# Half of the first batch's decay matrices from device memory instead of TensorE

## The reference, cut to what matters

```python
for t in range(S):
    m_new = np.maximum(f_gate[:, :, t] + m, i_gate[:, :, t])
    f_stab = np.exp(f_gate[:, :, t] + m - m_new)
    i_stab = np.exp(i_gate[:, :, t] - m_new)
    m = m_new
    C = f_stab[:, :, None, None] * C + i_stab[:, :, None, None] * np.einsum('bhd,bhe->bhde', vt, kt)
    n = f_stab[:, :, None] * n + i_stab[:, :, None] * kt
    h_tilde = np.einsum('bhde,bhe->bhd', C, qt)
    nq = np.einsum('bhd,bhd->bh', n, qt)[:, :, None]
    y[:, :, t] = sigmoid(o_gate[:, :, t]) * h_tilde / np.maximum(np.abs(nq), 1.0)
```

## Time and profile before

| what | value |
|---|---|
| median of 3 runs | 456.21 us (454.49 to 457.3) |
| the profiled execution's own time | 455.49 us |
| its span, first to last instruction | 453.8 us |
| mean granted TensorE clock | 0.995 |
| busy: TensorE / its weight loads | 439.6 us (97%) / 407.6 us (90%) |
| busy: VectorE, ScalarE, POOL | 255.6 (56%), 209.1 (46%), 208.3 (46%) us |
| chain that ended last | PE 85%, DVE 5%, issue 4%, ACT 4%, DMA 1% |
| moved by DMA | 47.38 MB, mean 104 GB/s over the span |

### The profile page before, as it was taken

One profiled execution on the slowest core, in us unless ns is written; L12 is line 12 of the kernel. 1 busy time (PEld: TensorE's weight loads), 2 busy tenths in 40 slices (PEclk: granted clock), 3 DMA queues, 4 the chain that ended last, 5 costly groups with the idle time before them and its releaser, 6 DMA issues.

```text
span 453.8 us, 9518 instructions
## 1 busy us (share of the span) xinstructions
PE 439.6 (97%) x3463; PEld 407.6 (90%) x3463; DVE 255.6 (56%) x592; ACT 209.1 (46%) x517; POOL 208.3 (46%) x293
## 2 busy tenths in 40 slices
PE   8899999999999999899999999999999999999996
PEld 3588988999999989799999998899999998999996
DVE  7689865777765356776674237666665326213122
ACT  3666459666554247654552137655652213211120
POOL 7535421789886333888861204798883000000000
PEclk9899999999999999999999999999999999999999
DMA  7557990443344415434454013534310010000101
GB/s 211 195 168 217 348 263 27 119 129 111 103 131 146 127 43 166 143 92 131 124 154 143 1 44 102 150 120 142 126 61 1 1 43 2 0 1 0 46 1 43
DMA packets 36616, 47.38 MB, mean 104 GB/s; under 512 B 3356, under 2 KB 29082, under 8 KB 36570
## 3 DMA queue, kind: packets, MB, share of 16 engines
q1 hardware_dynamic: 35674, 45.76, 33.4%
q10 hardware_dynamic: 896, 1.02, 0.6%
HBM read 42.73 MB, written 4.03 MB: 103 GB/s over the span
## 4 chain that ended last, share of the span: by engine, by line
PE 85%; DVE 5%; issue 4%; ACT 4%; DMA 1%; DVEq 0%; POOL 0%; POOLq 0%; ACTq 0%
PE pC L1165 32%; PE pA L1236 7%; PE pA L1237 7%; PE pA L1238 7%; PE pS L1077 6%; PE pA L1165 5%; PE pY L1134 4%; PE pA L1240 3%; PE pA L1241 3%; PE pC L1015 2%; PE pY L1113 2%; PE pN L1089 2%; DVE gb L856 1%; PE pA L1195 1%; DMA x<-o_gate_dram 1%
## 5 line engine op out<-in xcount | busy, mean ns | idle before, releaser
L988 DVE SCALAR_TENSOR_TENSOR h_lo<-pA,h_hi 128x384 fp32r<-128x384 f32 x96 | 53.5, 557 | 147.9 <-ACT h_hi L760 147.9
L760 ACT ACTIVATE h_hi<-pA 128x384 fp32r<-128x384 f32 x96 | 46.8, 488 | 138.7 <-PE pA L1241 138.6
L1165 PE MATMUL pC<-wc_hi,h_hi 128*128 128x320 f32 x288 | 94.1, 327 | 1.1 <-DVE wc_lo L846 1.0
L1165 PE MATMUL pC<-wc_lo,h_hi 128*128 128x320 f32 x288 | 88.7, 308 | 0.0
L1165 PE MATMUL pC<-wc_hi,h_lo 128*128 128x320 f32 x288 | 88.4, 307 | 0.0
L494 POOL TENSOR_TENSOR gb<-gb,pb 128x384 f32<-128x384 f32 (+1 forms) x54 | 49.1, 909 | 63.9 <-ACT pb L628 63.4
L1236 PE MATMUL pA<-uT_hi,wc_hi 128*128 128x384 f32 x192 | 65.2, 340 | 0.3 <-DVE wc_lo L846 0.3
L1237 PE MATMUL pA<-uT_lo,wc_hi 128*128 128x384 f32 x192 | 64.7, 337 | 0.0
L1238 PE MATMUL pA<-uT_hi,wc_lo 128*128 128x384 f32 x192 | 64.3, 335 | 0.0
L1165 PEld LDWEIGHTS pC<-wc_hi,h_hi 128*128 128x128 f32 x288 | 54.0, 188 | 2.3 <-DVE h_lo L988 1.3
L1165 PEld LDWEIGHTS pC<-wc_lo,h_hi 128*128 128x128 f32 x288 | 54.2, 188 | 0.1
(11 more groups left out here) (135 smaller groups left out, 881.6 us busy)
## 6 DMA issues: line engine op xcount, KB each, us to landing
gb<-g_dram SPq DMA_DIRECT2D x18, 512.0 KB, 3.9
kv<-kvN_dram SPq DMA_DIRECT2D x24, 324.0 KB, 4.0
kd<-kT_dram SPq DMA_DIRECT2D x24, 180.0 KB
qz<-qT_dram SPq DMA_DIRECT2D x72, 60.0 KB
out_dram<-u SPq DMA_DIRECT2D x24, 160.0 KB, 1.9
qd<-qT_dram SPq DMA_DIRECT2D x20, 180.0 KB, 2.6
gq<-g_dram SPq DMA_DIRECT2D x45, 60.0 KB
wc_raw<-w_ch_dram SPq DMA_DIRECT2D x6, 384.0 KB, 6.1
```

Of the source, the lines that this page charges most:

```text
L760: nc.scalar.activation(h2[0][:, slot % 2], pA[slot % 2][:, 0:HALF], ACT.Relu).then_inc(h2_hi, 1)
L988: nc.vector.scalar_tensor_tensor(h2[1][:, slot % 2], pA[slot % 2][:, 0:HALF], 0.0, h2[0][:, slot % 2].bitcast(F32), ALU.max, ALU.subtract) ...
L1165: ins = mm(dst, a[p], b[q], start=first and n == 0, stop=last and n == 2)
```

## The change

In the first batch, the decays of chunks 3, 4 and 5 (`FIRST_LOADED` = 3) come the way that the later batches' do. `spread_decays` is left out for steps 9 to 17; the query decays are still spread by TensorE. SyncE stores G right behind the scores load of chunk 2, waits until both stores are complete, and loads the decays of chunks 3, 4 and 5, each as soon as the values product of the chunk that used the buffer is through. Loads around them change places: the rest of chunk 2 comes behind the stores, and the scores loads of chunks 3 and 4 come a place earlier relative to the rest of the chunk before. POOL masks each loaded chunk behind the scaling of the queries of the chunk before. ScalarE's `first_exps` waits for the mask and works in place in SBUF. A semaphore of its own, `first_masked`, counts these masks, and `decay_loads` counts the loads of the first batch too.

```diff
+FIRST_LOADED = 3
...
+        first_masked = sem("first_masked")
...
         def decay_loads(ba, c):
 
-            return (ba - 1) * (NC // Q) + c // Q + 1
+
+            return ba * (NC // Q) + c // Q + 1 - FIRST_LOADED // Q
...
             for n in range(4):
                 load_weight(n)
-            load_chunk(0, 2)
-            load_weight(4)
-            load_chunk(0, 3)
-            load_weight(5)
+            load_scores(0, 2)
             sp.wait_ge(g_ready, len(SEGMENTS))
             g_rows = G_row.rearrange("p (c t) -> p c t", t=L)
             sp.dma_start(g_dram[:, 0:NH, :].rearrange("c p t -> p c t"), g_rows).then_inc(g_out, 16)
             sp.dma_start(g_dram[:, NH:NH + 1, :].rearrange("c p t -> p c t"), g_rows[0:1]).then_inc(g_pad_out, 16)
-            load_chunk(0, 4)
+            load_rest(0, 2)
+            load_weight(4)
+            sp.wait_ge(g_out, 16)
+            sp.wait_ge(g_pad_out, 16)
+            load_decays(0, 3)
+            load_scores(0, 3)
+            load_decays(0, 4)
+            load_rest(0, 3)
+            load_weight(5)
+            load_scores(0, 4)
+            load_decays(0, 5)
+            load_rest(0, 4)
             load_weight(6)
             load_chunk(0, 5)
             for n in range(7, NW):
                 load_weight(n)
-            sp.wait_ge(g_out, 16)
-            sp.wait_ge(g_pad_out, 16)
             for c in range(R):
                 load_chunk(1, c)
...
                 for g in range(NG):
                     tile = gb[:, r, GH * g:GH * g + HEADS[g], :]
+                    done = g_masked if ba > 0 else first_masked
                     nc.gpsimd.affine_select(out=tile, in_=tile, compare_op=ALU.is_ge, fill=NEG, base=0,
-                                            pattern=[[0, HEADS[g]], [1, L]], channel_multiplier=-1).then_inc(g_masked, 1)
+                                            pattern=[[0, HEADS[g]], [1, L]], channel_multiplier=-1).then_inc(done, 1)
...
                     if c < NC - 1:
                         weigh(0, c)
                     scale_q(0, c)
+                    if FIRST_LOADED <= c + 1 < NC:
+                        mask(0, c + 1)
                     if c >= 3:
                         x_low(0, c - 3)
...
                 c, g = divmod(m, NG)
                 if g == 0:
                     act.wait_ge(aT_ready, segment(c))
-                    if c >= Q:
-                        act.wait_ge(y_mm, NG * (c - Q + 1))
-                act.wait_ge(g_mm, m + 1)
+                if c < FIRST_LOADED:
+                    act.wait_ge(g_mm, m + 1)
+                else:
+                    act.wait_ge(first_masked, m - NG * FIRST_LOADED + 1)
                 for j in range(HEADS[g]):
                     head = GH * g + j
-                    last = nc.scalar.activation(gb[:, c % Q, head, :], pA[m % 2][:, j * L:(j + 1) * L], ACT.Exp,
+                    tile = gb[:, c % Q, head, :]
+                    sums = pA[m % 2][:, j * L:(j + 1) * L] if c < FIRST_LOADED else tile
+                    last = nc.scalar.activation(tile, sums, ACT.Exp,
                                                 bias=aT[:, c, bass.ds(head, 1)])
                 last.then_inc(e_exp, 1)
...
                         if k < STEPS:
-                            spread_decays(k)
+                            if k < NG * FIRST_LOADED:
+                                spread_decays(k)
                             if k == 2:
                                 keep_warm(WARM_THIRD)
```

## The result

The kernel got slower by 3.3%: 470.23 us (468.76 to 472.49, six runs) against 455.62 (454.00 to 457.30, six runs beside them), ratio 1.033 [1.030, 1.036]. The prediction was 459.2, with 456.0 to 463.0 as its range, and it was wrong.

The account below looks back on a forecast made before the run. VectorE's queue was taken to bound the first batch's attention for 17.6 us. Its delay of 2.2 us, grown by 1.3 to 3.5, less 0.1 from TensorE, gave 455.5 + 3.4 = 458.9, with half the distance to the median 459.2; range 456.0 to 463.0.

Parts of the forecast that it names:

- The sum that gave 459.2: Whole kernel: profiled 455.5 us plus 3.4 of delay in the first batch's attention, plus half the distance to the median.
- TensorE falls to half clock in the stall: Rival, chance 0.20: TensorE idles 2.3 us in attention and its clock halves; 460.6 us with one dip, 462.0 with two.
- the first stall's 2.2: VectorE at the first weight split, started at 34.22 us before, waits 2.2 us for ScalarE, done at 36.45.
- TensorE's queue was full up to the stall: Argument against the half-clock rival: ahead of the earlier dip, before 12.93 us, TensorE had only small products.
- First decay load: Chunk 3's decays on SyncE's queue: issued at 26.7 us, landed at 32.0, first mask part ready at 32.5.
- Its use at 33 us leaves about 1 us: Chunk 3's moved scores load (keys and queries) goes out 0.5 us later than 26.7, with about 1 us to spare.
- the forecast's 4.4: Landing time in us taken for values issued right behind a decay load, in place of 3.3 without one.
- ScalarE's queue and VectorE's first stall: Three steps' exponentials stand ahead of the first weight split: ScalarE needs 3.94 us, done at 36.45; VectorE stalls 2.2.
- Chunks 4 and 5: Later loads in attention: second split ready at 42.4 us, covered by 0.1; third at 49.9, delay growing to 3.5.
- the forecast's second stall: VectorE at the third weight split waits about 1.4 us for ScalarE; the delay grows by 1.3.
- What goes: Nine steps' spreading products leave TensorE, 2.7 us of work; worth 0.3 at most, since only step 6's is on the chain.
- the forecast's 3.4: Delay in us at 51.57, the first dense product: 3.5 from VectorE's stalls less 0.1 given back by TensorE.

Follow-up runs that it names:

- before_with_stall: The kernel before with one added wait: step 9's scores wait for weight 5 to land, no added transfer; 475.99, 465.30, 474.64 and 466.79 us against 455.27.
- gap_filled: The kernel after with 12 fillers (TensorE products of constants that nobody reads) ahead of step 9's scores; 469.51 us against 455.27, 1.031.
- scores_first: The kernel after with SyncE issuing chunk 3's keys and queries ahead of that chunk's decays; 470.91 us, 1.035.
- splits_and_scores_early: scores_first with ScalarE's halves of the early weight splits three steps sooner, ahead of the exponentials that wait for POOL; 468.73 us against 454.67, 1.029.
- all_filled: The kernel after with 55 fillers (products nobody reads), ahead of steps 9 and 17 and behind the scores of steps 10 to 16; 462.95 us, 1.018.
- spread_kept: The kernel after with the spreading products of steps 9 to 17 put back on TensorE, their sums unused; 473.12 us, 1.040.
- loads_only: The kernel before with SyncE's new order and three decay loads that nobody reads; 470.44, 464.76, 472.29 and 458.89 us against 454.46.
- filled_lean: The kernel after with 29 fillers (products nobody reads), fewer than all_filled; 470.40, 458.48, 462.52 and 461.45 us, without the slowest 1.014.
- spread_left_out: The kernel before without the spreading products of steps 9 to 17, nothing in their place; ten runs, 452.88 to 467.52 us against 454.46, the seven lower 1.001.
- stall_filled: before_with_stall with 18 fillers (products nobody reads) on TensorE ahead of the added wait; 457.17 us against 454.67, 1.005.
- splits_early_filled: splits_and_scores_early with 33 fillers (products nobody reads) behind the scores of steps 9 to 17; 466.37, 459.90, 465.30 and 461.39 us, 1.018.

## Why the prediction was wrong, point by point

**The step that failed.** The sum that gave 459.2 has no term for the clock: it took the stage to run at full clock but for one chance in five. And the rival that had the clock, "TensorE falls to half clock in the stall", mis-sized its one term: "in a dip of 3.3 us it gets through 0.97 of a step where VectorE would have gone 1.65: 1.4 us each". The rival's mechanism was right, and so was its 3.4 us a step at half clock (measured 3.0 to 3.4 up to step 15). The length was not: the dip lasted 34 us, and with it the way from step 9 to the dense part took 12.6 us more (the table above). The 3.3 us were taken from the earlier trace rows, the only dip that the trace of before had, as if its length were a constant. In attention it is not: in *before_with_stall* one idle time of 3.90 us brought 41 us. With a dip up to the dense part the rival would have stood near 470 (estimate: 455.5, the first stall's 2.2, and nine steps at 3.36 instead of 2.0 us), and a range that held it at 0.20 could not have ended at 463.0.

**Its chance** was too low as well. "TensorE's queue was full up to the stall" counted against it; before the stall that *gap_filled* left, too, TensorE had been busy, and the clock fell all the same. The Trainium skill (TensorE: Matmul & The Clock Gate, "HAM oscillation — how this bites in real kernels") was the warning, and it spoke for the right case; the traces agree that idle times between bursts bring the fall. The Trainium skill (TensorE: Matmul & The Clock Gate, "Part 1: The HAM clock gate") puts the penalty of the ramp at a kernel's start under 1% of a typical span; that is no price for a fall in the middle, behind which the stage here ran up to 12.6 of 467 us longer (2.7%).

**First decay load.** Landed at 31.95 (24.95 + 7.0) against 32.0. The two errors cancel: it went out 1.75 us earlier than 26.7, as the whole start was earlier in this execution, and took 7.0 us instead of 5.3. The first mask ran at 32.10, in 0.47 us each (1.41 for three).

**"Its use at 33 us leaves about 1 us"**, of chunk 3's keys and queries, failed: they were in at 33.60, 6.11 us after the last issue, and TensorE, with its start 1.75 earlier and the early spreading products gone, wanted them at 31.08. I had given the new load's bytes to the decays alone, and not to what stands behind it: values of chunk 3 took 7.2 us instead of the forecast's 4.4, the weight 8.3 where the one of the same place took 4.2 before. (The values landed at 36.4, where 36.3 was forecast, but by two errors: issued 2.7 us sooner, 2.8 longer under way.) The burst's DMA share of 1.00 lasted until 36 us. This put TensorE's idle time at 31.1 us instead of 35.8, and on the queries instead of VectorE; *scores_first* shows that the total hardly depends on it (the +3.1 and +12.6 of the table became +1.1 and +15.0).

**ScalarE's queue and VectorE's first stall.** Right in kind and place: 36.64 against 36.45. The wait was 3.90 instead of 2.2, because VectorE came to it 1.5 us sooner (32.77 against 34.22) and the split was 0.2 later; as the rest of the start was 1.8 us sooner, the agreement of 36.64 is in part luck. *splits_and_scores_early* took this wait away, and the time hardly moved.

**Chunks 4 and 5.** The times at full clock agree to 0.2 us (*all_filled*, 42.32 and 49.94), but mostly by luck: the first split stood at 35.52 there, so that from it to the third it took 14.4 us and not 13.5, with fillers and longer landings in it, and the forecast's second stall, VectorE's for ScalarE at the third split, is in no trace at more than 0.24 us. Where the clock stood at 1.00 ahead of 47 us (*spread_kept*, *loads_only*, *filled_lean*), the second gap was TensorE's own, 2.2 to 2.3 us, at the state product that waits for POOL's weighting of chunk 4. In the kernel after there is no second gap: behind the fall TensorE was busy up to the dense part but for 0.14 us.

**What goes.** Right as far as the times can tell: 0.25 of 2.7 us in one trace (*spread_left_out*).

**Where the loss came from.** The loads make TensorE wait, at one of three places (queries of chunk 3; VectorE behind ScalarE's queue; values of chunk 3 or 4 behind POOL); an idle time of 2 to 4 us lets the clock fall; and attention then runs at half clock until the dense part. In the kernel before, such a stall is worth 2.5 us by itself, and 10 to 21 with the fall (*stall_filled*, *before_with_stall*). For the change itself the share is bounded only: of its 14.6 us at least 6.3 are the clock's, since with the fillers in it and no fall it stands at 8.3 (*all_filled*), and some 8 to 11 by the runs of *filled_lean* at 0.999 and 1.000. That any one of the gaps is enough is shown by taking others away; that the fall costs more than the stall is shown by the pair of stalls with and without fillers.

**What stays open.** The cost of this change at full clock was not measured free of fillers: *all_filled* bounds it above by 8.3 us, the runs of *filled_lean* at 0.999 and 1.000 stand at +4.0 and +7.0, and the one of *loads_only* at 1.000, which has the loads alone, at +4.4. All lie above the forecast's 3.4, with fillers or the spreading products in them, so it is neither confirmed nor excluded. Why the clock came back after 3.4 us in the first falls of *spread_kept* and *loads_only* and in other falls not for 20 to 41 us, is not explained either. No version of the change that was tried beats the kernel before.

## What to carry to other kernels

In a stage where TensorE has small products and little reserve, price a stall in two parts: its own length, and what the work up to the next dense stretch costs at half clock; the second was the larger one here (2.5 us without the fall, 10 to 21 with it). Don't take the length of one dip in the trace as that of the next. An added load is paid for by the transfers issued behind it on the same queue as much as by its own landing, so give each of them the longer landing and look up who wants it. And before removing work from TensorE where it is off the critical path, ask whether it was what kept the clock; here that is likely, not shown.

## What the runs showed of the hardware

- Half clock can outlast its cause by far. By the profile TensorE had no idle time any more (3.00 of 3 us in 63 to 66), and still the clock stayed at 0.50 until the dense products had run for 2.4 us. (The ends of matmuls are modelled, so that short gaps between them wouldn't show.) In the seven profiled executions in which gaps were left (the kernel after, *gap_filled*, *scores_first*, *spread_kept*, *before_with_stall*, *splits_and_scores_early*, *loads_only*) the last fall lasted 20 to 41 us and ended 2.4 to 5.1 us into the dense part. In *splits_early_filled*, with fillers in every step, it ended after 10 us, within attention.
- The mean granted clock of a run tells the time at half clock without a trace: (1 - 0.963) x 2 x 467.3 = 34.6 us, where the stretches gave 34.1. All six runs of the kernel after lie at 0.956 to 0.963.
- The clock can fall when TensorE has already begun again: 1.3 us after the gap in *gap_filled* (38.84, 40.1), 1.6 in *filled_lean* (47.69, 49.3), 0.5 in *loads_only* (48.05, 48.6).
- In the profiled runs, up to 80 us, all eleven idle times of 1.96 to 4.27 us in attention were followed by a fall. The gap that ends near 13 us was followed by one in *before* (1.86 us), *spread_kept* and *spread_left_out* (1.93), and by none in *loads_only* (1.88), *filled_lean* (1.87) and *stall_filled* (1.90), at nearly the same length.
- The fall is a matter of chance in some kernels. *loads_only* gave 458.89 and 472.29 us for the same program on the same chip, at clocks of 1.000 and 0.959.
- Eighteen products that nobody reads saved 8 to 19 us (*stall_filled*, 457.17, against the four runs of *before_with_stall*, 465.3 to 476.0).
- Behind a 512 KB load on the same queue, chunk 3's values (324 KB), its queries (180 KB) and the next weight (384 KB) took 7.2, 7.6 and 8.3 us to land instead of 3.3, 3.3 and 4.2, at a DMA share of 1.00.
